# Another place in SBUF for the four read passes of a matmul's moving rows, and results written to PSUM in address order

## What is computed

```python
x, f_logit: (2, 6080, 256)   lower_bound: (256,)   w_in: (256, 2048)   w_out: (2048, 256)
sig = 1.0 / (1.0 + np.exp(-f_logit))
f = lower_bound[None, None, :] + (1.0 - lower_bound[None, None, :]) * sig
i = 1.0 - f
for t in range(S):
    h = f[:, t] * h + i[:, t] * x[:, t]
    y[:, t] = h
h = y.reshape(B * S, D) @ w_in
g = np.where(h > 0.0, h, np.exp(np.minimum(h, 0.0)) - 1.0)
return (g @ w_out).astype(np.float32)
```

## Time and profile before

| | us |
|---|---|
| median of 3 runs | 961.75 |
| lowest and highest of them | 961.59, 965.25 |
| the profiled execution, its own time | 962.05 |
| span of its records | 960.2 |
| PE busy in the span | 954.3 |
| ACT busy | 790.1 |
| DVE busy | 722.3 |
| POOL busy | 628.8 |

### The profile page before, as it was taken

One profiled execution on the slowest core, in us unless ns is written; L12 is line 12 of the kernel. 1 busy time (PEld: TensorE's weight loads), 2 busy tenths in 40 slices (PEclk: granted clock), 3 DMA queues, 4 the chain that ended last, 5 costly groups with the idle time before them and its releaser, 6 DMA issues.

```text
span 960.2 us, 15016 instructions
## 1 busy us (share of the span) xinstructions
PE 954.3 (99%) x4362; PEld 815.4 (85%) x4362; DVE 722.3 (75%) x916; ACT 790.1 (82%) x1424; POOL 628.8 (65%) x477
## 2 busy tenths in 40 slices
PE   9999999999999999999999999999999999999998
PEld 6999888888888888888888888888888888888887
DVE  6998876976886796697688679679768867966444
ACT  7989888878888888888888888888888788887775
POOL 2578796576667668557656755856775765676544
PEclk9999999999999999999999999999999999999999
DMA  7212012002101201100210210120021021001001
GB/s 273 68 33 95 0 34 66 34 1 78 55 1 55 77 1 44 55 33 1 75 55 0 66 66 0 45 66 20 23 65 44 0 76 55 0 0 46 1 1 45
DMA packets 23078, 42.02 MB, mean 44 GB/s; under 512 B 2560, under 2 KB 4096, under 8 KB 23040
## 3 DMA queue, kind: packets, MB, share of 16 engines
q1 hardware_dynamic: 22752, 41.10, 13.2%
q10 hardware_dynamic: 288, 0.46, 0.1%
HBM read 29.10 MB, written 12.45 MB: 43 GB/s over the span
## 4 chain that ended last, share of the span: by engine, by line
PE 96%; ACT 2%; DVE 1%; issue 1%; POOL 0%; ACTq 0%; POOLq 0%
PE acc L896 17%; PE acc L898 17%; PE acc L897 17%; PE h L868 14%; PE h L866 14%; PE h L867 14%; ACT e L472 1%; PE h L1010 1%; PE h L1002 1%; PE h L1004 1%; PE h L1003 1%; ACT e L466 1%; DVE x L628 0%; PE h L968 0%; ACT w_out_hi L505 0%
## 5 line engine op out<-in xcount | busy, mean ns | idle before, releaser
L336 POOL TENSOR_TENSOR g_lo<-e,g_hi 128x512 fp32r<-128x512 f32 (+1 forms) x384 | 516.4, 1355 | 325.5 <-ACT g_hi L480 324.0
L466 ACT ACTIVATE e<-h 128x512 f32<-128x512 f32 (+1 forms) x379 | 224.8, 593 | 124.6 <-PE h L868 90.3
L719 DVE SCALAR_TENSOR_TENSOR e<-e,h 128x512 f32<-128x512 f32 (+1 forms) x379 | 256.8, 678 | 70.2 <-ACT e L472 69.1
L896 PE MATMUL acc<-g_hi,w_out_hi 128*128 128x512 f32 (+1 forms) x768 | 291.1, 379 | 0.4 <-DVE w_out_lo L690 0.4
L898 PE MATMUL acc<-g_hi,w_out_lo 128*128 128x512 f32 (+1 forms) x768 | 291.0, 379 | 0.0
L897 PE MATMUL acc<-g_lo,w_out_hi 128*128 128x512 f32 (+1 forms) x768 | 290.9, 379 | 0.0
L472 ACT ACTIVATE e<-e 128x512 f32<-128x512 f32 (+1 forms) x384 | 241.3, 628 | 9.7 <-issue 1.2
L480 ACT CAST g_hi<-e 128x512 fp32r<-128x512 f32 (+1 forms) x384 | 232.1, 604 | 19.3 <-DVE e L719 19.3
L866 PE MATMUL h<-a_hi,w_in_hi 128*128 128x512 f32 x616 | 234.7, 381 | 0.0
L868 PE MATMUL h<-a_hi,w_in_lo 128*128 128x512 f32 x616 | 234.7, 381 | 0.0
L867 PE MATMUL h<-a_lo,w_in_hi 128*128 128x512 f32 x616 | 234.7, 381 | 0.0
(11 more groups left out here) (77 smaller groups left out, 556.0 us busy)
## 6 DMA issues: line engine op xcount, KB each, us to landing
opening<-forget_logit SPq DMA_DIRECT2D x44, 256.0 KB, 2.7
x<-value SPq DMA_DIRECT2D x44, 256.0 KB, 2.7
out<-out_sb SPq DMA_DIRECT2D x44, 256.0 KB, 2.0
w_in_raw<-w_in SPq DMA_DIRECT2D x8, 256.0 KB, 5.4
w_out_raw<-w_out SPq DMA_DIRECT2D x8, 256.0 KB, 6.5
out<-out_sb SPq DMA_DIRECT2D x4, 224.0 KB, 1.9
x<-value SPq DMA_DIRECT2D x3, 224.0 KB, 6.1
opening<-forget_logit SPq DMA_DIRECT2D x2, 224.0 KB, 6.3
```

The source lines that it names most:

```text
L336: nc.gpsimd.tensor_tensor(g_lo[:, t % RING, 0:w], e[:, t % TILES, 0:w], g_hi[:, t % RING, 0:w].bitcast(F32), ALU.subtract).then_inc(g_lo_r ...
L466: nc.scalar.activation(e[:, i, 0:w], bank_of(j, t)[:, 0:w], ACT.Relu, scale=-1.0).then_inc(r_ready, 1)
L719: nc.vector.scalar_tensor_tensor(e[:, t % TILES, 0:w], e[:, t % TILES, 0:w], -1.0, bank_of(j, t)[:, 0:w], ALU.add, ALU.max).then_inc(g_rea ...
L896: nc.tensor.matmul(bank, hi, g_h, start=opens, stop=False)
```

## The change

A new function `in_passes` describes a row by pass, run and column: a pass begins 40 columns (ten lines of 16 bytes) after the one before it, its runs of 8 columns are 32 columns apart. Column n of the row's content, counted in the order in which this pattern visits it, is token n. The matmuls read the rows by this pattern and write their PSUM bank from its first column on. So a row must be stored by the same pattern: ACT's rounding copies write by it, and the subtractions of POOL and DVE read their hi row and write their lo row by it, their other input lying as before.

A row then reaches 96 columns past its 512, into places that the pattern leaves free in the next row. All hi and lo rows of both layers move into one tensor `rows` in which neighbours interlock; `ROW_OF` and `G_ROW` number them. The last four low parts of the plain weights lie over rows 1 to 4 in place of four of the old ones.

The matmuls of the first block that ran over 512 columns run over 448. The three memsets of POOL and `zeros_ready` are gone. One matmul of 64 columns (new L1004) is there that fills the last 64 columns of one bank before the blocks of 512 begin. Weights, the warm-up and the waits of the other instructions are as before.

```diff
+RUN = 8
+PASSES = 4
+PASS_STEP = 40
...
-def in_order(columns):
-
-    return columns.rearrange("p (b a c) -> p a b c", a=APART, c=LINE)
+def in_passes(row, w):
+
+    return bass.AP(row.tensor, row.offset,
+                   [row.ap[0], [PASS_STEP, PASSES], [PASSES * RUN, w // (PASSES * RUN)], [1, RUN]])
...
+        spill = (PASSES - 1) * (PASS_STEP - RUN)
+        rows = sb("rows", [P, ROWS * TILE + spill], F32R)
...
+        def row(n):
+            return rows[:, n * TILE:(n + 1) * TILE]
...
-                nc.gpsimd.tensor_tensor(g_lo[:, t % RING, 0:w], e[:, t % TILES, 0:w],
-                                        g_hi[:, t % RING, 0:w].bitcast(F32),
+                nc.gpsimd.tensor_tensor(in_passes(g_lo(t), w), e[:, t % TILES, 0:w],
+                                        in_passes(g_hi(t), w).bitcast(F32),
                                         ALU.subtract).then_inc(g_lo_ready, 1)
...
-            for part in (a_hi, a_lo):
-                nc.gpsimd.memset(part[:, 0, P1:P2 + 1, SHORT:TILE].bitcast(F32), 0.0).then_inc(zeros_ready, 1)
-            nc.gpsimd.memset(a_hi[:, 0, P5, SHORT:TILE].bitcast(F32), 0.0).then_inc(zeros_ready, 1)
...
-                nc.scalar.copy(g_hi[:, t % RING, 0:w], e[:, t % TILES, 0:w]).then_inc(g_hi_ready, 1)
+                nc.scalar.copy(in_passes(g_hi(t), w), e[:, t % TILES, 0:w]).then_inc(g_hi_ready, 1)
...
-                into = in_order(bank[:, 0:w])
-                a_h, a_l = in_order(a_h[:, 0:w]), in_order(a_l[:, 0:w])
+                into = bank[:, 0:w]
+                a_h, a_l = in_passes(a_h, w), in_passes(a_l, w)
...
-                bank, g_h, g_l = in_order(bank), in_order(g_h), in_order(g_l)
+                g_h, g_l = in_passes(g_hi(t), w), in_passes(g_lo(t), w)
...
+                    nc.tensor.matmul(bank, hi, a_h, start=half == 0, stop=False)
                     if t == TILES * PAIRS - 2 and half == 0:
 
-                        nc.tensor.matmul(in_order(h[:, 3]), hi, in_order(a_parts(0, P5)[0]), start=True, stop=False)
-                    else:
-                        nc.tensor.matmul(bank, hi, a_h, start=half == 0, stop=False)
+                        nc.tensor.matmul(h[:, 3, SHORT:TILE], hi, in_passes(a_parts(0, P5)[0], TILE - SHORT),
+                                         start=False, stop=False)
```

More of the change, by code:

```diff
@@ L50 @@
               + [(1, 2, 3, 0)[t % TILES] for t in range(UNITS)])
+ROW_OF = {}
+for _part in range(2):
+    for _n, _product in enumerate((P3, P6, P7, P1, P2, P5)):
+        ROW_OF[0, _product, _part] = (0 if _n < 3 else 3) + _n + 3 * _part
+        ROW_OF[1, _product, _part] = 14 + _n + 6 * _part
+    ROW_OF[0, P4, _part] = ROW_OF[1, P4, _part] = 12 + _part
+G_ROW = 26
+ROWS = G_ROW + 2 * RING
 QUARTER = ((P1, P5), (P2, P3))
 PLACE = ((P1, P2), (P5, P4))
-def in_order(columns):
-    return columns.rearrange("p (b a c) -> p a b c", a=APART, c=LINE)
+def in_passes(row, w):
+    return bass.AP(row.tensor, row.offset,
+                   [row.ap[0], [PASS_STEP, PASSES], [PASSES * RUN, w // (PASSES * RUN)], [1, RUN]])
 def width(j):
@@ L116, in gated_scan_elu_ffn @@
         x = sb("x", [P, BATCH, HALVES, TILE])
[L117 to L125, removed]
+        spill = (PASSES - 1) * (PASS_STEP - RUN)
+        rows_at = -(-nc.sbuf_base // 32) * 32
+        rows = sb("rows", [P, ROWS * TILE + spill], F32R)
+        for p in range(PAIRS // 2, PAIRS):
+            w_plain_low.append(nc.alloc_sbuf_tensor_at(f"w_plain_lo{p}", [P, 4, P], F32R,
+                                                       offset=rows_at + 4 * TILE * (p - PAIRS // 2 + 1)))
         e = sb("e", [P, TILES, TILE])
         p5 = sb("p5", [P, TILE])
-        g_hi = sb("g_hi", [P, RING, TILE], F32R)
-        g_lo = sb("g_lo", [P, RING, TILE], F32R)
         carry = sb("carry", [P, BATCH, HALVES, 1])
@@ L197, in plain_done, with g_hi, g_lo @@
             return max(t for t in range(TILES * PAIRS) if FIRST_TILES[t][1] // 2 == p) + 1
+        def row(n):
+            return rows[:, n * TILE:(n + 1) * TILE]
         def a_parts(par, product):
[L200 to L203, removed]
+            return row(ROW_OF[par, product, 0]), row(ROW_OF[par, product, 1])
+        def g_hi(t):
+            return row(G_ROW + t % RING)
+        def g_lo(t):
+            return row(G_ROW + RING + t % RING)
         def y(b, i, w):
@@ L960, in first_products @@
             def first_products():
-                pieces = [a_parts(0, PLACE[0][i]) for i in range(HALVES)]
-                pe.wait_ge(zeros_ready, 3)
+                pieces = [[in_passes(part, SHORT) for part in a_parts(0, PLACE[0][i])] for i in range(HALVES)]
                 for half in range(HALVES):
@@ L967, in first_products @@
                         pe.wait_ge(w_plain_hi_ready, unit // 2 + 1)
-                        nc.tensor.matmul(in_order(first_bank(unit)), plain_weights(unit, half)[0],
-                                         in_order(pieces[half][0]), start=half == 0, stop=False)
+                        nc.tensor.matmul(first_bank(unit)[:, 0:SHORT], plain_weights(unit, half)[0],
+                                         pieces[half][0], start=half == 0, stop=False)
                 for unit in range(OPEN):
-                    w = TILE if unit < WIDE else SHORT
-                    bank = in_order(first_bank(unit)[:, 0:w])
+                    bank = first_bank(unit)[:, 0:SHORT]
                     if unit == 0:
                         pe.wait_ge(a_lo_ready[P1], 1)
-                    nc.tensor.matmul(bank, plain_weights(unit, 0)[0], in_order(pieces[0][1][:, 0:w]),
+                    nc.tensor.matmul(bank, plain_weights(unit, 0)[0], pieces[0][1],
                                      start=False, stop=False)
@@ L978, in first_products @@
                     for half in range(HALVES):
-                        nc.tensor.matmul(bank, plain_weights(unit, half)[1], in_order(pieces[half][0][:, 0:w]),
+                        nc.tensor.matmul(bank, plain_weights(unit, half)[1], pieces[half][0],
                                          start=False, stop=False)
@@ L982, in first_products @@
                         pe.wait_ge(a_lo_ready[P2], 1)
[L983 removed]
+                    done = nc.tensor.matmul(bank, plain_weights(unit, 1)[0], pieces[1][1],
                                             start=False, stop=True)
```

17 lines of the change are left out of this document (6 added, 11 removed).

## The result

The changed kernel takes 1016.87 us (median of 4, 1016.22 to 1017.44) against 961.85 us before: 1.0564 times, 95% interval 1.0545 to 1.0583. It is slower by 55 us, where 953 was forecast.

The account below looks back on a forecast made before the run. The prediction took the distance between PE's matmul starts as the bound. From the profiled 962.05 us it took 8.7 for writing PSUM in one run and 0.27 for the opening: 953.1, stated as 953.0 against the median, range 942 to 968.

Parts of the forecast that it names:

- What bounds the kernel: From 45.90 us on, the distance between PE's matmul starts alone was said to set the end, over 95% of the span.
- A hop between runs costs nothing: In PE's reading and writing, jumps between runs were called free: fp32r surplus 6.7 ns at 512 columns, 6.9 at 448.
- paid once per matmul or once per pass: PE's 4.3 ns of fp32r surplus above bf16 was put down to number type or pass starts in reading or writing.
- Writing PSUM in one run: At PE's fp32r matmuls, a gain of 2.1 ns each, 8.7 us in all; bounds 0 and 17.9 us.
- The split of the 4.3 ns: PE's fp32r surplus above bf16 was divided evenly between reading and writing, 2.1 ns taken for the writing.
- Ten lines between the passes: PE's longer hop between reading passes, in place of two lines: zero taken, with a loss of up to 10.7 ns possible.
- The slower rival: New pass starts meet weight loads or other readers at each PE matmul: 5.3 ns, 983.8 us; chance 0.15.
- The stores: Short-run row stores by ACT, POOL and DVE: zero taken, 1.0 us kept for ACT before 45.9 us.
- The rival of feeders: Stores hold up the engines feeding PE, POOL needing 2.03 us per operation in place of 1.36; chance 0.03.
- The opening: First-block matmuls of 448 columns in place of 512 bring the result ACT waits for earlier: a gain of 0.27 us.
- The range: 942 to 968 us for the whole kernel, leaving out mostly the slower case's larger prices.
- The Trainium skill's rule on PSUM: Non-contiguous PSUM access slows matmuls significantly; it supported the rival giving writing the whole surplus: 943.9 us, chance 0.19.

Follow-up runs that it names:

- e5: The kernel before with the weights 32 bytes further in SBUF and every row where it was: 989.37 us, ratio 1.0276.
- e6: The kernel before with the weights and all rows 32 bytes further in SBUF, together: 961.86 us, ratio 0.9995.
- e8: The changed kernel with the weights 128 bytes further in SBUF and all rows where they were: 1024.76 us, ratio 1.0654.
- e1: The changed kernel with pass starts 8 columns apart in place of 40, the rest of the change kept: 961.6 us, ratio 0.9994.

## Why the prediction was wrong, point by point

- **What bounds the kernel** was read rightly: the end is the distance of PE's starts times 4158, to 1% (the stretch is 94.9% of the span, not quite the "over 95%" of the text). So 13 ns became 54 us.
- **"A hop between runs costs nothing"** rested on one surplus at two widths (6.7 at 512 and 448). It was true of that one arrangement. With passes 40 apart the surplus is 20.0 at 512 and 16.9 at 448, and rows in one run, without a hop, have 13.4 at 512 and 20.0 at 448. From a flat line at one pattern the prediction went on to "paid once per matmul or once per pass", and there the argument left the trace.
- **Writing PSUM in one run: 2.1 ns taken, 0 measured.** This is the first term that failed. The split of the 4.3 ns between reading and writing was a guess between three candidates; the stretches show nothing of it on the write side (L97 and L99 alike) and none of it with bf16 (L133 as fast as L130). The bf16 rows were called the nearest ones for the write side; they differ in the element's type as well, and that was the part that counted.
- **Ten lines between the passes: 0 taken, +13.3 ns measured**, beyond the upper bound of 10.7. This is the term that decided. The text named the mechanism (reads that meet the weight loads) and had a row for it: the earlier trace rows show PE slower by 10 to 11 ns with no wait and full clock. It chose zero because "the steady rows are nearer"; but they are nearer only to the old step, for which no row of a new one stood in. Nor need be a disturbance from outside. In the matmuls alone, with no other engine at work, 448 columns in passes 8 apart show both distances; these are the first 11 and the last 32 of one stretch:

```profile
230.22 2.40 PE L125 MATMUL banks<-rows,wt 128*128 128x448 f32 x11
235.75 6.35 PE L125 MATMUL banks<-rows,wt 128*128 128x448 f32 x32
```

(2.40 - 0.36) / 10 = 0.204 us, then (6.35 - 0.36) / 31 = 0.193. So the earlier trace rows read as a second distance of the old pattern, and that was no bound for the new one.
- **The slower rival** had the right mechanism and place, 0.15 as its chance and 5.3 ns as its price. At 13.3 ns it gives 962.05 + 55.3 - 0.27 = 1017.1, the time that came out. Its condition "meets the weight loads or the other readers" is settled against the other readers, since with the other engines silent the distance is the same, and for the weight loads by e5, e6 and e8, where only the place of the weights against the rows changed the time.
- **The stores** cost nothing, as taken: copies 605 ns, subtractions 1361, and e1 has the time of before. The rival of feeders falls.
- **The opening**: ACT's first L472 starts at 12.12 us in place of 12.69, 0.57 earlier against 0.27 forecast; some of it is the earlier end of the wait for ACT's copy. "ACT is the chain from there on" no longer held: PE, slower at 448 columns too, never waits after 10 us and takes the gain back (46.70 in place of 45.91 us, above). In e1, where PE is not slower, the whole time is that of before, so that nothing of the 0.27 us can be told from the noise.
- **The range** left out "mostly the larger prices of the slower case"; that is where the time fell. The Trainium skill's rule on PSUM, one of the rivals' supports, pointed to a gain too.

What stays open: the mechanism in the hardware. Shown is that the distance depends on the place of weights and rows to each other and on the step of the passes (8, 72 and 136 columns, 256 bytes apart, are the only ones that reached 220.0; 136 was run once), that it does not depend on how PSUM is written, in the patterns tried, or on other engines, and that it takes steady values which persist. Not shown is what is shared by the two readings, why fewer weight columns do not help, what picks between two distances, and why four timings of the kernel before took 965.0 to 965.3 us, between them.

## To carry to other kernels

A PE-bound kernel with fp32r operands has a layout term: the same instructions took 961.9 us or, with the weights 32 bytes further, 989.4. Before such a pattern or an address is changed, time it in a stretch of matmuls alone, beside the old one, with several entries. And when a trace shows an engine slower at full clock without a wait, as the rows after the wait did here, a change that touches what this engine reads may bring the cause back; a zero for it needs its own measurement.

## What the runs showed of the hardware that was not expected

- With fp32r, matmuls of 512 columns started 220.0, 226.7, 230.7 or 233.3 ns apart in the kernels above, 235.4 in e8, and up to 246.6 in matmuls alone, by address and pattern; with bf16 it was 215.8 to 216.0, in the patterns tried.
- The Trainium skill says in "TensorE: Matmul & The Clock Gate", Step-by-step: what each phase is for, that PE has two independent read ports and that loading the next weights doesn't steal SBUF read bandwidth from the running matmul. For fp32r these runs speak against the second part: moving only the weights cost 27.5 us, moving weights and rows together cost nothing.
- One and the same program has two steady distances, 220.0 and 230.7 ns. The traced execution that went over to 230.7 at 88 us kept it for the 914 us that were left.
